# Block-sparse attention and two mixtures of experts: the logit sums in a scatter of their own, half of the list columns on ACT, one function set, and a later output copy

## What is computed

```python
# attention: a window of 16 tokens around each token, and block summaries (max of k, mean of v)
a = softmax(concat([masked q.k, q.k_sum + log(32)])); x = a @ concat([v, v_sum])
# first mixture: noisy scores, the two best experts of each token
noisy = x @ w_gate + log1p(exp(x @ w_noise)) * noise
for e in range(E):
    for k in range(2):
        mask = top2[:, k] == e
        out[mask] += top2_w[mask, k, None] * (np.maximum(x[mask] @ w1[e], 0.0) @ w2[e])
# second mixture on the first one's output: skip where x @ w_skip <= 0, else the single best expert
out = x.copy()
out[do_compute] = xc + gate_w * (np.maximum(xc @ w1[e], 0.0) @ w2[e])
```

## Time and profile before

| | us |
|---|---|
| median of 3 runs | 697.66 (695.53 to 697.94) |
| the profiled execution | 695.7, span 693.9 |
| attention, to the last router logits | 0 to 110.5 |
| first routing and first gather, to the first product of round 0 | 110.5 to 142.96 |
| first mixture, 8 rounds | 142.96 to 467.1 |
| turning x1, second routing, first gather | 467.1 to 503.5 |
| second mixture, 14 slots | 505.2 to 681.8 |
| last scatter and end | 681.8 to 693.9 |

### The profile page before, as it was taken

The page is one execution under the profiler, slowest core; times in us unless marked ns, Lnnn a source line. Parts: engine busy times, 40 slices in busy tenths (PEclk is TensorE's granted clock), DMA queues, the critical chain, the costliest instruction groups (busy, mean ns, idle before and its releaser), DMA issues.

```text
span 693.9 us, 13641 instructions
## 1 busy us (share of the span) xinstructions
PE 633.5 (91%) x4142; PEld 562.3 (81%) x4142; DVE 381.4 (55%) x742; ACT 293.2 (42%) x503; POOL 206.9 (30%) x225
## 2 busy tenths in 40 slices
PE   6688883799999999999999999998699999999993
PEld 6576773489999999999999999986478888788882
DVE  3686787645363545446355544531665677656731
ACT  2365662043253444334243433424164575545620
POOL 1538860220241506033240604203023233131230
PEclk9999997599999999999999999999799999999997
DMA  9999995126182744719272562788546769568130
GB/s 225 205 254 258 265 308 205 47 85 212 51 230 73 179 145 104 237 52 260 64 202 106 135 209 61 221 300 207 164 154 202 224 197 340 165 183 262 32 59 1
DMA packets 98034, 119.39 MB, mean 172 GB/s; under 512 B 57444, under 2 KB 57700, under 8 KB 97968
## 3 DMA queue, kind: packets, MB, share of 16 engines
q1 hardware_dynamic: 80432, 94.04, 44.2%
q0 software_dynamic: 10464, 23.83, 16.0%
q10 hardware_dynamic: 7072, 0.73, 0.7%
HBM read 103.24 MB, written 23.34 MB: 182 GB/s over the span
## 4 chain that ended last, share of the span: by engine, by line
PE 75%; SPq 8%; DVE 5%; DMA 4%; issue 3%; ACT 1%; POOL 1%; POOLq 0%; DVEq 0%; ACTq 0%
PE bank L845 21%; PE bank L839 21%; PE bank L952 19%; SPq L520 5%; SPq L535 2%; PE bank L828 2%; PE bank L808 2%; PE bank L737 1%; PE bank L968 1%; DMA out<-y_sb,ix_put 1%; PE bank L720 1%; PE bank L749 1%; DVE col_val L1702 1%; PE bank L709 1%; DMA xg<-x_moe,ix_take 1%
## 5 line engine op out<-in xcount | busy, mean ns | idle before, releaser
L1544 DVE TENSOR_TENSOR w_lo<-stage,w_hi x120 | 141.6, 1223 | 22.5 <-ACT w_hi L1076 21.9
L1076 ACT CAST w_hi<-stage x120 | 119.6, 1047 | 9.6 <-PE bank L952 9.5
L845 PE MATMUL bank<-unit_hi,w_hi 128*128 128x416 f32 x256 | 92.6, 362 | 0.0
L1795 DVE SCALAR_TENSOR_TENSOR unit_lo<-bank,unit_hi 128x416 fp32r<-128x416 f32 x64 | 37.9, 592 | 97.2 <-ACT unit_hi L1162 97.2
L839 PE MATMUL bank<-tok_hi,w_hi 128*128 128x416 f32 x256 | 90.6, 354 | 0.7 <-DVE bank L1830 0.7
L845 PE MATMUL bank<-unit_lo,w_hi 128*128 128x416 f32 x256 | 90.2, 352 | 0.0
L839 PE MATMUL bank<-tok_hi,w_lo 128*128 128x416 f32 x256 | 89.7, 350 | 0.0
L845 PE MATMUL bank<-unit_hi,w_lo 128*128 128x416 f32 x256 | 89.7, 350 | 0.0
L1162 ACT ACTIVATE unit_hi<-bank 128x416 fp32r<-128x416 f32 x64 | 33.2, 519 | 130.2 <-PE bank L839 130.2
L1366 POOL DMA_INDIRECT x_moe<-rows_out,ix_put x32 | 59.0, 1844 | 57.8 <-DVE rows_out L1783 36.2
L839 PE MATMUL bank<-tok_lo,w_hi 128*128 128x416 f32 x256 | 58.5, 350 | 0.0
(11 more groups left out here) (170 smaller groups left out, 1086.4 us busy)
## 6 DMA issues: line engine op xcount, KB each, us to landing
stage<-in_moe_w SPq DMA_DIRECT2D x128, 512.0 KB, 5.7
v_win<-in_v SPq DMA_DIRECT2D x24, 192.0 KB, 5.9
x_moe<-rows_out SPq DMA_DIRECT2D x12, 260.5 KB, 4.6
x_att<-x_sb POOLq DMA_DIRECT2D x12, 256.0 KB, 4.6
x_part<-x_moe SPq DMA_DIRECT2D x4, 768.0 KB, 8.9
rows_in<-x_part SPq DMA_DIRECT2D x12, 256.0 KB, 4.0
out<-x_moe SPq DMA_DIRECT2D x4, 768.0 KB, 8.7
late_raw<-in_v SPq DMA_DIRECT2D x6, 384.0 KB, 7.0
```

What stands on the lines that cost most here:

```text
L845: last = eng.matmul(ps_out[chunk][:, 0:W], w[:, WC // 2 + f, chunk * P:(chunk + 1) * P], h[:, f % UNITS, :], start=(f == 0 and i == 0), st ...
L1076: eng.copy(piece(w_hi[n % SETS], j), stage[:, j, :]).then_inc(s_hi, 1)
L1544: eng.tensor_tensor(piece(w_lo[n % SETS], j), stage[:, j, :], piece(w_hi[n % SETS], j).bitcast(F32), ALU.subtract)\
L1795: eng.scalar_tensor_tensor(unit_lo[:, f % UNITS, :], ps_unit[f % 2][:, 0:W], 0.0, unit_hi[:, f % UNITS, :].bitcast(F32), ALU.max, ALU.subt ...
```

## The change

1. `x_moe` rows shrink from 521 to 520 elements. The 9 logit sums go to a tensor of their own, `x_more`, by four more accumulating scatters in each `put`, issued ahead of the four of the rows. They wait for a new semaphore `s_sums`, which DVE raises in block 1 of the next round. `x_more` is zeroed by one more DMA. The second router reads its first group after the eighth sums have landed, ahead of SP's last `x_part` tile, no longer after `s_m1done`.
2. ACT makes `lane_hot` for every second pick of the first router and of the second group of the second (`by_act`, 12 and 3 picks), with two instructions each: the square of (lane - column), then relu(1 - square).
3. ACT loads the function set that holds exponential and logarithm once, at the start.
4. `out`'s copy waits until the first gather of the second mixture has landed.
5. On PE: `ps_more` is cleared before the first filler matmuls of round 0, which now wait for it (`s_last_gates`); no filler ahead of the fourth part; part 0 is turned in another bank; 2 filler matmuls ahead of the last `turn_y`, 3 ahead of the first x1 tile; the ranks of the second router's first group come one tile later and ahead of that tile's products.
6. `xt_hi` is rounded in two halves, each with its own signal, and PE starts on the first. ACT's first store of the second gates comes after all tiles and after `s_m1done`.

```diff
@@ SP @@
             eng.wait_ge(round_sems["xtp"],
                         eng.snap(total, min_val=0, max_val=E * ROUNDS) * PARTS + (PARTS + 1))
...
             for t in range(NT):
+                if t == NT - 1:
+
+                    all_rounds = eng.snap(total, min_val=1, max_val=E * ROUNDS)
+                    for part in range(PARTS):
+                        eng.wait_ge(s_put_sums[part], all_rounds * 16)
+                    load_sums(0)
                 if t >= XR:
                     eng.wait_ge(s_x1t, t - XR + 1)
...
+            load_sums(1)
+            land(0)
             eng.wait_ge(s_m1done, 1)
...
-            land(0)
+
+            eng.wait_ge(slot_sems["take"], 16)
             for rows in base_rows:
@@ PE @@
+                eng.wait_ge(s_last_gates, 2)
                 keep_warm(12, ps_turn)
                 for t in range(PARTS):
                     eng.wait_ge(s_take[t], 16)
-                    turn_x(0, t, ps_out[t])
-                    keep_warm(3, ps_turn)
-                eng.wait_ge(s_last_gates, 2)
+                    turn_x(0, t, ps_first[t])
+                    keep_warm(0 if t == PARTS - 2 else 3, ps_turn)
...
+                keep_warm(2, ps_unit[0])
                 turn_y(eng.snap(number, min_val=0, max_val=E * ROUNDS), 0, logits=True)
...
-                        eng.wait_ge(S["xth"], sv + 1)
-                        products(ps_h[0], up[0], 0, H)
+                        eng.wait_ge(S["xth"], sv * 2 + 1)
+                        products(ps_h[0], up[0], 0, H // 2)
+                        eng.wait_ge(S["xth"], sv * 2 + 2)
+                        products(ps_h[0], up[0], H // 2, H)
...
+            keep_warm(3, ps_unit[0])
             eng.wait_ge(s_xt_idle, 1)
...
+                if t == first[1] + 4:
+                    ranks(1, first)
                 if 1 <= t <= NT:
                     eng.wait_ge(s_x1te, t)
                     second_logits(t - 1)
                 if t >= 2:
                     turn_logits(t - 2)
-                if t == first[1] + 3:
-                    ranks(1, first)
@@ ACT @@
+            eng.preload_act_table_set("natural_log_exp_and_others")
...
+                def nearness(at):
+                    eng.wait_ge(s_far, by_act.index(at) + 1)
+                    eng.activation(lane_hot[at % HR][:], lane_hot[at % HR][:], ACT.Relu, scale=-1.0,
+                                   bias=1.0).then_inc(s_near, 1)
+
+                for i, at in enumerate(mine):
+                    t, pick = divmod(at - 2 * m * NT, picks)
+                    if at >= HR:
+                        eng.wait_ge(s_list, at - HR + 1)
+                    eng.activation(lane_hot[at % HR][:], lane_h[:], ACT.Square, scale=-1.0,
+                                   bias=lane_f[:, pick, t:t + 1]).then_inc(s_far, 1)
+                    if i:
+                        nearness(mine[i - 1])
+                nearness(mine[-1])
@@ POOL, put @@
+                    eng.wait_ge(s_sums, n + 2)
+                    eng.wait_ge(S["ix"], n + 1)
+                    eng.sem_inc(S["start"], 1)
+                    for t in range(PARTS):
+                        rows = PART[t]
+                        eng.indirect_dma_start(more_dram,
+                                               bass.IndirectOffsetOnAxis(ap=ix_put[0:rows, t:t + 1],
+                                                                         axis=0),
+                                               more_out[0:rows, t, :], None, bounds_check=N - 1,
+                                               oob_is_err=False, compute_op=ALU.add)\
+                           .then_inc(s_put_sums[t], 16)
                     eng.wait_ge(S["ye"], n * DK + (DK + 2))
-                    eng.wait_ge(S["ix"], n + 1)
@@ DVE, lists @@
-                        eng.tensor_scalar(lane_hot[at % HR][:], lane_h[:], lane_f[:, i, t:t + 1],
-                                          None, ALU.is_equal)
+                        if at not in by_act:
+                            eng.tensor_scalar(lane_hot[at % HR][:], lane_h[:], lane_f[:, i, t:t + 1],
+                                              None, ALU.is_equal)
@@ DVE, round @@
                                 if e == E - 1:
                                     logits(n, dn)
+                                else:
+                                    eng.sem_inc(s_sums, 1)
```

More of the change, by code:

```diff
@@ L309, in build @@
         xt_hi, xt_lo = [sb_in(routing, f"xt_{part}", [P, DK, P], F32R) for part in ("hi", "lo")]
-        xg = sb_in(routing, "xg", [P, D + LOGITS])
+        xg = sb_in(routing, "xg", [P, ROW])
         y_sb = sb_in(routing, "y_sb", [P, D])
@@ L320, in build @@
         out_t = sb_in(rounds, "out_t", [P, W])
-        rows_out = sb_in(rounds, "rows_out", [P, PARTS, D + LOGITS])
+        rows_out = sb_in(rounds, "rows_out", [P, PARTS, ROW])
         rounds.close()
@@ L383, in build @@
         s_may_put = sem("s_may_put")
+        s_sums = sem("s_sums")
+        s_put_sums = [sem(f"m0_put_sums{t}") for t in range(PARTS)]
         s_last_gates = sem("s_last_gates")
@@ L393, in build @@
             "xtp": "PE: they are transposed (one more than slots)",
-            "xth": "ACT: rounded, in xt_hi",
+            "xth": "ACT: rounded, one more half of them in xt_hi",
             "xte": "DVE: the rest is in xt_lo",
@@ L500, in build @@
         group_no = {mg: i for i, mg in enumerate((m, g) for m in range(2) for g in GROUPS[m])}
+        by_act = [2 * t + 1 for t in range(NT)] + [2 * NT + t for t in range(GROUPS[1][1][0], NT, 2)]
         block = keep.enter_context(nc.Block())
@@ L792, in lists @@
                     eng.wait_ge(s_hot, at + 1)
+                    if at in by_act:
+                        eng.wait_ge(s_near, by_act.index(at) + 1)
                     eng.matmul(ps_list[:, 0:NCOL], lane_hot[at % HR][:], col_val[at % HR][:],
@@ L1118, in store_gates, with lanes @@
                    .then_inc(s_gates, 16)
+            def lanes(m, group):
+                eng.wait_ge(s_lane, group_no[m, group] + 1)
+                t0, t1 = group
+                picks = (2, 1)[m]
+                mine = [at for at in by_act if picks * t0 <= at - 2 * m * NT < picks * t1]
+                def nearness(at):
[11 more added lines that the diff above has]
+                nearness(mine[-1])
             def empty_x1(t):
@@ L1203, in round_x @@
                     eng.wait_ge(S["xtp"], n + (ahead + 2))
-                    eng.copy(xt_hi[:].rearrange("p k n -> p (k n)"), ps_xt[:]).then_inc(S["xth"], 1)
+                    for i in range(0, DK, 2):
+                        eng.copy(xt_hi[:, i:i + 2, :].rearrange("p k n -> p (k n)"),
+                                 ps_xt[:, i * P:(i + 2) * P]).then_inc(S["xth"], 1)
                 j = eng.alloc_register(f"act_piece{m}")
@@ L1248, in _ @@
             store_gates(0, GROUPS[0][0])
+            lanes(0, GROUPS[0][0])
             first_mixture()
@@ L1256, in _ @@
                     weights(1, first)
-                if t == first[1] + 4:
-                    store_gates(1, first)
+            eng.wait_ge(s_m1done, 1)
+            store_gates(1, first)
             weights(1, second)
             store_gates(1, second)
+            lanes(1, second)
             second_mixture()
@@ L1689, in route @@
                 eng.scalar_tensor_tensor(lane_f[:, mine, tiles], block_f[:, mine, tiles], float(-P),
-                                         near[:, mine, tiles], ALU.mult, ALU.add)
+                                         near[:, mine, tiles], ALU.mult, ALU.add).then_inc(s_lane, 1)
                 then(eng.tensor_tensor(col_f[:, mine, tiles], block_f[:, mine, tiles],
@@ L1765, in logits @@
                         rows = PART[t]
-                        last = eng.tensor_scalar(rows_out[0:rows, t, D:D + LOGITS],
+                        last = eng.tensor_scalar(more_out[0:rows, t, :],
                                                  ps_more[0:rows, t * LOGITS:(t + 1) * LOGITS],
                                                  gates_last[0:rows, t:t + 1], None, ALU.mult)
-                    return last
+                    last.then_inc(s_sums, 1)
                 def columns(n, chunk):
@@ L1827, in first_mixture @@
                 for t in range(PARTS):
-                    rest_of_x(0, t, ps_out[t])
-                eng.wait_ge(S["xte"], PARTS + 1)
-                eng.memset(ps_more, 0.0).then_inc(s_last_gates, 1)
+                    rest_of_x(0, t, ps_first[t])
                 for e in range(E):
@@ L1852, in rest_of_x @@
                 def rest_of_x(ahead, n):
-                    eng.wait_ge(S["xth"], n + (ahead + 1))
+                    eng.wait_ge(S["xth"], n * 2 + (2 * ahead + 2))
                     if ahead:
```

28 lines of the change are left out of this document (20 added, 8 removed).

## The result

| | before | after |
|---|---|---|
| median of 10 runs each, us | 696.62 (693.92 to 700.10) | 699.37 (698.15 to 701.77) |
| the profiled execution | 695.7, span 693.9 | 698.5, span 696.7 |

The account below looks back on a forecast made before the run. PE, busy 91% of the span, was taken as the bound, with gains only where it waits, in the two routings. Terms -1.3 - 2.0 - 0.5 + 0.1 - 1.7 + 3.2 - 0.3 = -2.5 took 697.66 to 695.2 us; range 691.0 to 699.5.

Parts of the forecast that it names:

- Part 1: First routing: ACT's table load between exponential and logarithm lies on the only chain, so removing it gives -1.3 us.
- Part 2, first router: First router's lists: DVE saves 12 of 24 `lane_hot` at 0.17 us and still sets the pace, -2.0 us.
- Second router: Second router's last group: three `lane_hot` leave DVE at 0.17 us each, -0.5 us.
- Part 3: Start of round 0: fillers wait for `ps_more` +1.4, against 0.7 and 0.6 back; +0.1 us, bounds -1.3 and +1.4.
- Part 4, the chain to x1: Round 7 to x1: four small scatters delay the rows' landing and the `x_part` copy by 3.8 us; PE +3.2.
- my first rival: The copy to `x_part` is not late: part 4 is -1.0 instead of +1.5, sum -5.0, 692.7 us; chance 0.32.
- the last rival: Scatters held up, 2.85 us each: copy to `x_part` 9.9 us late, x1 tiles +9.3, 701.3 us; chance 0.10.
- SP's copy to `x_part` waits for that landing: After round 7: the copy, starting at 446.11, waits for the scatter landing at 444.3, so it moves by 3.8 us.
- Part 4, ranks: Second routing: ranks one tile later give PE 1.7 us of work during its 1.71 us mask wait, -1.7.
- Part 5, 0 for the second gather: Slot 0: 1.8 us of cover remain for the second gather, so 0; landing in 9.6 us, PE loses 1.1.
- my second rival: ACT or the output copy eats the gain: slow ACT pairs 697.2, or second gather stalls PE 696.3; chance 0.13.
- `xt_hi`, -0.3: Second mixture's first product: PE waits 0.68 us for `xt_hi`; half the width is ready some 0.3 us sooner.

Follow-up runs that it names:

- the lists alone: The kernel before with one function set, ACT's share of `lane_hot` and `xt_hi` in halves, no new tile or DMA; 690.55 us, ratio 0.9936.
- the set alone: The kernel before with only the early load of the function set for exponential and logarithm added; 693.58 us, ratio 0.9957.
- trimmed kernel: Changed kernel, `more_out` placed last, without the later output copy, the fillers' wait for `ps_more` and the 2 and 3 new fillers; 691.17 us, ratio 0.9927.
- kernel with `more_out` at the end: The changed kernel with its new tile `more_out` moved behind `rows_out`, so earlier tiles lie where they lay before; 693.73 us, ratio 0.9975.
- the eight profiles: Profiles of the kernel before and the seven runs whose `stage` begins at a multiple of 256 bytes; exponential at 108.1 to 111.9 us.
- the six: Profiles of the six other runs, whose `stage` does not begin at a multiple of 256 bytes; exponential at 112.7 to 118.8 us.

## Why the prediction was wrong, point by point

**What bounds the kernel.** I took attention, 110 us, as untouched because no instruction in it changed. Its loads keep the DMA engines busy throughout, and the place of their target was changed. This is the step that failed for the total, and it isn't even in the text: the sum has no term for the new tile. It is worth +6 (6.55 in the two profiles, ratio 1.0086 for a like tile alone), and alone makes the forecast wrong.

**Part 1, -1.3: right.** The removed load is 1.29 us on the row, and 32.47 - 30.95 = 1.5 us for the stage.

**Part 2, first router -2.0: right.** 9.16 to 7.21 us on PE; 30.95 to 29.14 = -1.8 for the stage. ACT's pair takes 0.69 us, issued every 0.61: above my 0.62, below the 0.8 at which it would have cost. **Second router -0.5: right.** From the ranks of the second group to `take_ix` it takes 5.67 us in all eight profiles in which DVE makes every `lane_hot`, 5.19 with the lists alone, and 5.30 in the five kernels with the whole change. From x1 to slot 0 it is hidden, 37.27 us with the set alone and 37.26 with the lists, because other parts of that way differ by as much from profile to profile.

**Part 3, +0.1: too small.** 29.77 and 29.85 us against 29.14 are +0.7. The trimmed kernel shows the two parts of it: the fillers' wait for `ps_more` costs 1.5 (28.30), near my upper bound of 1.4, and the earlier clearing, the other bank and the missing group of fillers give 0.8 back, not 1.3.

**Part 4, the chain to x1, +3.2: wrong; my first rival was right.** The four small scatters took a little less than I said, 1.61 us on average against 1.76 (those of whole rows 1.73 in after), so nothing of the last rival, with 2.85 us for each; and the rows' first starts 9.1 us behind DVE's sums, 6.8 later than before (forecast 7.5). But the copy to `x_part` came only 1.5 us later against the sums (19.85 us behind them, 18.35 before), not 3.8: before, it had waited for weight pieces, whose loads the change does not touch. The failed step is "SP's copy to `x_part` waits for that landing"; SP's own waits, which I had not read, show it, and my own sum had a sign of it: it put the landing at 444.3, 1.8 us ahead of the copy at 446.11. And the 1.5 us are gone before the x1 tiles, since the pieces behind the copy land after 7.4 us of waiting instead of 10.0. The small slack was right, 0.6 us at most in my text and 0.4 us of SP's wait for PE in both profiles; nothing used it up. What remains are the 5 new fillers, +0.5 to +0.6, which the trimmed kernel loses again.

**Part 4, ranks, -1.7: wrong.** The wait is 1.79 us, 1.71 before. I put DVE's start by SP's issue; the reads of 27 KB landed 2.5 us after their issue before, and 5.7 beside the scatters of the rows (medians of two). Where the first landed sooner, after 4.4 us in the trimmed kernel, PE's wait was 0.41 us.

**Part 5, 0 for the second gather: wrong.** It landed in 9.9 us, near the 9.6 of my bound. PE waited 1.1 to 2.1 us in all three kernels with the copy at this place, as in my second rival. The same move let ACT's two stores of gates land in 2.0 us each instead of 8.7 and 3.7, which gained nothing against before, since no gather waited for them there. **`xt_hi`, -0.3: right**; the wait fell from 0.68 to 0.46 us.

**The sum.** x1 to slot 0 takes 37.3 to 39.7 us in nine profiles of kernels with the old order, 38.3 on average, and 36.6 to 36.8 in three with the changed one; so profiles of one run each leave this term between -1.1 and -1.7. Part of it is in no term of mine: PE's turn of the first gathered rows takes 1.05 us in before, where the granted clock is at half until 504.7, and 0.60 in after. Without attention the terms measured are -1.5 - 1.8 + 0.7 + 0.6 - 1.4 + 1.5 (slots, 176.5 against 175.0 on average) - 0.9 (the end) = -2.8. The kernel with `more_out` at the end is 2.3 us faster by the medians. That the forecast of these parts was -2.5 is luck: of its eight terms three were off by more than a microsecond, in both directions. Some small sums were off too, without weight for the forecast: four pieces issued at 452.3 that land 14.5 us later land at 466.8, not 466.6; three gaps shortened from 2.34 to 1.9 us give 1.3 back, not 1.4; the refill has 457.4 - 444.3 = 13.1 us of room, not 12.5; and 692.7 less 1.96 is 690.7, not 691.0. The 0.9 us at the end, seen in every kernel with the change's `x_more` and in none without, I can't explain: the last scatter is issued a microsecond later behind the last products there, and the end still comes sooner.

## What to carry to other kernels

When a change adds or resizes a tile, list the addresses before and after and ask which DMA targets moved; in a stage bound by loads of 256-byte pieces, keep the target's start at a multiple of 256 bytes, or put the new tile last. Before a step is taken to wait for the one ahead of it, read the waits of its own queue: the one that ends last may be another transfer. The large copy delayed the small transfers beside it; moving it chose which one, and at the best of its three places it still cost one wait of 1.3 us.

## What the runs showed of the hardware that I had not expected

- Packets of 256 bytes took 18.4 to 19.0 ns of an engine where their target began at a multiple of 256, and 25.0 to 26.4 where it began 32, 128, 160 or 192 bytes past one, whatever the distance. The loaded weights, in pieces of 2 KB and more, showed nothing of it: from 200 to 400 us a packet of 2048 bytes took 89.3 to 93.2 ns on average in the eight profiles and 89.7 to 93.4 in the six.
- An accumulating scatter of 128 rows of 36 bytes kept POOL nearly as long as one of 2080 bytes: at the least 1.56 us for both in after, 1.33 for both with 32 rows, and 1.61 and 1.73 us on average over all four parts.
- With the 3 MB copy of the output issued ahead of them, two stores of 24 KB landed in 7.2 to 9.9 and in 2.8 to 7.6 us; with the copy behind them, in 1.9 to 2.0.
- Behind a wait of 2.5 us PE's granted clock was at half (1.2 instead of 2.4 GHz) for 3.4 us, and the slot took 1.5 us longer.
